# The product q (kᵀv) as two 64-row tiles of the TensorE array, in an fp32 attention + two-layer MoE kernel on one core

## The chip, the cores and the metric

The program runs on 1 core of one Trainium2 chip. Its time is the device time of that core in microseconds (us). It was timed three times before the change; "median" is the median of these. A further execution was recorded by the profiler, and all rows below are from it.

## The reference

Three blocks follow one another on 2304 tokens (4 batches of 576) and a width of 512 (8 heads of 64):

```python
kv  = einsum('bhsd,bhse->bhde', k, v)            # 64x64 per batch and head
out = einsum('bhsd,bhde->bhse', q, kv)
x   = out / sqrt(mean(out*out, -1) + 1e-6) * g_norm      # then heads side by side: x is [2304, 512]

h = x @ w_in ; x = (max(h,0) + alpha*min(h,0)) @ w_out    # d_ff 2048

P = exp(x @ w_gate - max) ; 8 times: rows / sum, columns / sum, * N/E
y = sum over 8 experts e of P[:, e] * (max(x @ w1[e], 0) @ w2[e])    # d_ff 1024 each
```

All inputs and the output are float32. The change lies wholly in the second einsum and what reads its result; it keeps the values.

## The kernel before, in words

Each of the five engines has an instruction list of its own, written out by hand; the order in a list is the order in time, and lists meet only at semaphores (`wait_ge`, `then_inc`). No planner is involved. TensorE is PE below, VectorE DVE, ScalarE ACT, GpSimd POOL, SyncE SP.

**Attention** is worked in 16 turns (`TURNS`), one for each batch and pair of heads (h = 0, 1). The 576 tokens of a turn lie as 96 partitions times 6 tokens (`ROWS`, `TG`), and are taken in pairs: an even token (o = 0) and the odd one after it (o = 1). For turn n:

- SP loads q, k and v (288 KB each) into one of four buffer sets (`load_qkv`, L352). From turn 4 on it first waits for `kv_done` of the turn four before. The weights of the first MoE unit are loaded behind turn 5, those of the next two behind turn 15 (L368, L373).
- PE `turn_q` (L926): 6 transposes bring q to qT, for each (h, t) a block of 128 rows (even token's 64 dimensions above, odd one's below) by 96 columns. ACT `take_q` (L502) copies it from PSUM.
- PE `multiply_kv` (L941): kᵀv, summed for even tokens in PSUM rows 0 to 63 and for odd ones in rows 64 to 127. Each of its 12 matmuls (24 instructions, since fp32 goes in two passes) loads 64 columns and moves 64: two halves of the array by columns. It waits for `kv_in` and for `kvd_ready` of the turn before.
- ACT `take_kv` (L507) copies the two halves to `kvp`; PE `spread_kv` (L948) multiplies by the matrix `both`, which adds the halves and leaves the sum in both; DVE `take_kv` (L690) copies it to `kvd`.
- PE `multiply_q` (L958), for turn n in the PE list behind `multiply_kv` of turn n+1: 6 matmuls (12 instructions), stationary the 128 x 96 block of qT, moving the 128 x 128 block of `kvd`. `kvd` is block diagonal: kᵀv in two corners, zeros in the other two, so one matmul gives the outputs of an even and of an odd token. The zeros are written once by POOL (L418).
- ACT `squares` (L512) and DVE `square_sums` (L683) sum squares over 64; ACT `root` (L517), DVE `norm` (L696 reciprocal, L700 multiply) give the normalised `xs`; PE `turn_x` (L972), two groups of 3 transposes, and ACT `take_x` (L523), twice, bring it to `x` with the factor g_norm.

The PE list of a turn is: `turn_q(n)`, `turn_x(n-3, 0)`, `multiply_kv(n)`, `turn_x(n-3, 1)`, `multiply_q(n-1)`, `spread_kv(n)`. Both halves of `turn_x` write one PSUM bank, so the second waits until ACT has copied the first. The ACT list of a turn is `squares(n-2)`, `take_q(n)`, `take_x(n-3, 0)`, `root(n-2)`, `take_kv(n)`, `take_x(n-3, 1)`. `multiply_q` of turn 15 and the last `turn_x` stand among the first matmuls of the MoE blocks (`behind`). In the last turns (13 to 15) DVE also runs `factor_low` (L726), which splits x for the MoE blocks.

**The MoE blocks** run in 120 units on the same five engines; matmuls in fp32r with the operands split in high and low parts (L1050, L1052, L1053 the first product, L1078 to L1080 the second). Nothing of them is touched by the change.

Of the kernel before, what the change touches and what calls it, by code (L numbers as in the profile page):

```python
# [8 lines left out]
ALU = mybir.AluOpType  # L9
ACT = mybir.ActivationFunctionType  # L10
AX_X = mybir.AxisListType.X

P = 128
BATCH, HEADS, SEQ, DH = 4, 8, 576, 64
# [7 lines left out]
ROWS = 96  # L22
TG = SEQ // ROWS
# [40 lines left out]
def moe_program(nc, q, k, v, g_norm, w_in, w_out, alpha, w_gate, w1, w2, out):  # L64
    ctx = ExitStack()
    with ctx:
        cursor = [(nc.sbuf_base + 31) // 32 * 32]

        def sb(name, shape, dt, at=None):

            size = 4
            for n in shape[1:]:
                size *= n
            where = cursor[0] if at is None else at
            if at is None:
                cursor[0] += (size + 31) // 32 * 32
                assert cursor[0] <= nc.sbuf_usable_end, (name, cursor[0], nc.sbuf_usable_end)
            return nc.alloc_sbuf_tensor_at(name, shape, dt, offset=where)

        def sem(name):  # L80
            return ctx.enter_context(nc.semaphore(name))
# [17 lines left out]
        hh_at = cursor[0]  # L99
# [30 lines left out]
        BUFFER = 2 * TG * DH * 4  # L130
# [5 lines left out]
        def attention_buffers(at, **shapes):  # L136
            found = []
            for name, shape in shapes.items():
                found.append(sb(name, shape, F32, at=at))
                at += (4 * math.prod(shape[1:]) + 31) // 32 * 32  # L140
            return found

        qT, xs, kvp = attention_buffers(acc_at, qT=[P, 2, SEQ], xs=[ROWS, 2, TG, 2, DH], kvp=[P, 2, DH])
        sq, ssq, rms, rinv = attention_buffers(hh_at + 4 * BUFFER, sq=[ROWS, 2, TG, DH], ssq=[ROWS, 2 * TG],
                                               rms=[ROWS, 2, 2 * TG], rinv=[ROWS, 2 * TG])
        kvd, = attention_buffers(hh_at + 4 * BUFFER + 4096 + 2 * BUFFER, kvd=[P, 2, 2, P])
        alpha_rows = c22[0:MLP_SETS * 2 * CHUNKS, 0:P]

        ps = ctx.enter_context(nc.psum_tensor("ps", [P, 8, 512], F32))

        const_ready = sem("const_ready")
# [11 lines left out]
        kvd_ready = sem("kvd_ready")  # L163
# [5 lines left out]
        xs_ready = sem("xs_ready")  # L169
# [139 lines left out]
        def o_banks(n):  # L309
            return ps[0:ROWS, 2 * (n % 2):2 * (n % 2) + 2, 0:TG * DH]  # L310
# [93 lines left out]
        def _(pool):  # L404
            made = [0]

            def constant(instruction):
                made[0] += 1
                instruction.then_inc(const_ready, 1)
                pool.wait_ge(const_ready, made[0])  # L410

            def diagonal(m, base):
                constant(nc.gpsimd.affine_select(out=m, in_=m, compare_op=ALU.not_equal, fill=1.0, base=base,
                                                 pattern=[[-1, P]], channel_multiplier=1))

            constant(nc.gpsimd.memset(ident[:, :], 0.0))
            diagonal(ident[:, :], 0)
            constant(nc.gpsimd.memset(kvd[:, :, :, :], 0.0))  # L418
            constant(nc.gpsimd.memset(both[:, :], 0.0))
            for base in (0, DH, -DH):  # L420
                diagonal(both[:, :], base)
# [71 lines left out]
        def _(sc):  # L493
# [15 lines left out]

            def squares(n):  # L510
                sc.wait_ge(o_done, n + 1)
                nc.scalar.activation(sq[:, :, :, :].rearrange("p h t d -> p h (t d)"), o_banks(n), ACT.Square)\  # L512
                    .then_inc(sq_ready, 1)

            def root(n):
# [15 lines left out]
                nc.scalar.activation(high(s, i), whole(s, i), ACT.Copy).then_inc(xc_hi, 1)  # L531


            sc.wait_ge(const_ready, 8)
            nc.scalar.activation(unused[:, :], eps[:, :], ACT.Sqrt).then_inc(table_in, 1)
            for n in range(TURNS):
                if n >= 2:
# [78 lines left out]
            def step(u):  # L616
                s = stage_of(u) + 1
                splits = SPLITS_AT.get(before_last(u), ())
                if u == 0:
                    squares(TAIL_X + 1)  # L620
                    take_x(TAIL_X, 0)
                    take_x(TAIL_X, 1)
# [57 lines left out]
        def _(dve):  # L680
            def square_sums(n):
                dve.wait_ge(sq_ready, n + 1)
                nc.vector.reduce_sum(ssq[:, :], sq[:, :, :, :].rearrange("p h t d -> p (h t) d"), AX_X)\  # L683
                    .then_inc(ssq_ready, 1)

            def take_kv(n):
                dve.wait_ge(kv_spread, n + 1)
                for o in range(2):
                    r = slice(o * DH, (o + 1) * DH)
                    last = nc.vector.tensor_copy(  # L690
                        kvd[r, n % 2, :, r], ps[r, 6, 2 * P:2 * P + 2 * DH].rearrange("d (h e) -> d h e", h=2))
                last.then_inc(kvd_ready, 1)

            def norm(n):
                dve.wait_ge(rms_ready, n + 1)
                nc.vector.reciprocal(rinv[:, :], rms[:, n % 2]).then_inc(rinv_ready, 1)  # L696
                dve.wait_ge(rinv_ready, n + 1)
                if n >= 2:
                    dve.wait_ge(x_turned, 2 * (n - 1))
                nc.vector.tensor_tensor(  # L700
                    xs[:, n % 2].rearrange("p t h d -> p h t d"),
                    o_banks(n).rearrange("p h (t d) -> p h t d", d=DH),
                    rinv[:, :].rearrange("p (h t) -> p h t", h=2).unsqueeze(3).to_broadcast([ROWS, 2, TG, DH]),
                    ALU.mult).then_inc(xs_ready, 1)

            def factor_sum(s, i):

# [94 lines left out]
            spread = [P, GT, EXPERTS]  # L802
# [92 lines left out]
                        nc.vector.tensor_scalar(acc[:, t, :], acc[:, t, :], gate[:, t, 0:1], None, ALU.mult)\  # L895
                            .then_inc(gated, 1)

            dve.wait_ge(const_ready, 3)
            for n in range(TURNS):
                if n >= 2:  # L900
                    square_sums(n - 2)
# [14 lines left out]
        def _(pe):  # L916

            def turn_q(n):
                b, i = divmod(n, HEAD_PAIRS)
                qq = qkv[i][0].rearrange("p h (s o) d -> p h s (o d)", o=2)  # L920
                pe.wait_ge(q_in[i], 16 * (b + 1))
                if n >= 1:
                    pe.wait_ge(qT_ready, n)
                for h in range(2):
                    for t in range(TG // 2):
                        last = nc.tensor.transpose(ps[:, 4 + h, t * ROWS:(t + 1) * ROWS], qq[:, h, t, :],  # L926
                                                   ident[0:ROWS, 0:ROWS])
                last.then_inc(q_turned, 1)
# [16 lines left out]
            def spread_kv(n):  # L945

                pe.wait_ge(kvp_ready, n + 1)
                nc.tensor.matmul(ps[:, 6, 2 * P:2 * P + 2 * DH], both[:, :], kvp[:, :, :].rearrange("d h e -> d (h e)"),  # L948
                                 start=True, stop=True).then_inc(kv_spread, 1)

            def multiply_q(n):
                pe.wait_ge(qT_ready, n + 1)
                pe.wait_ge(kvd_ready, n + 1)
                if n >= 2:
                    pe.wait_ge(xs_ready, n - 1)
                for h in range(2):
                    for t in range(TG // 2):
                        last = nc.tensor.matmul(o_banks(n)[:, h, t * P:(t + 1) * P],  # L958
                                                qT[:, n % 2, (3 * h + t) * ROWS:(3 * h + t + 1) * ROWS],
                                                kvd[:, n % 2, h, :], start=True, stop=True)  # L960
                last.then_inc(o_done, 1)

            def turn_x(n, j):
                pe.wait_ge(xs_ready, n + 1)
                if n < TAIL_X:
                    pe.wait_ge(x_ready, 2 * n + j)
                else:
                    pe.wait_ge(qT_ready, TURNS)
                    if n > TAIL_X:
                        pe.wait_ge(x_ready, 2 * (n - 1) + j + 1)  # L970
                for t in range(TG // 2):
                    last = nc.tensor.transpose(x_bank(n, j)[:, t * ROWS:(t + 1) * ROWS], xs[:, n % 2, TG // 2 * j + t].rearrange("p h d -> p (h d)"),  # L972
                                               ident[0:ROWS, 0:ROWS])
                last.then_inc(x_turned, 1)

            pe.wait_ge(const_ready, 2)
            for n in range(TURNS):
                if n == 2:
                    pe.wait_ge(small_in, 64)
                    a = MLP_SETS * 2 * CHUNKS  # L980
                    nc.tensor.transpose(ps[:, 7, 0:a], alpha_rows, ident[0:a, 0:a]).then_inc(alpha_t, 1)
                if n == 3:
                    pe.wait_ge(alpha_ready, 1)
                turn_q(n)
                if n >= 3:
                    turn_x(n - 3, 0)
                if n == 0:
                    pe.wait_ge(const_ready, 7)
                multiply_kv(n)
                if n >= 3:  # L990
                    turn_x(n - 3, 1)
                if n >= 1:
                    multiply_q(n - 1)
                spread_kv(n)
# [121 lines left out]
            for u in range(UNITS + 1):  # L1116
                for i in range(PRODUCTS):
# [6 lines left out]
                    at = turn_at(u, i)  # L1124
                    if at:
                        turn_x2(*at)
                    at = logits_at(u, i)
# [22 lines left out]
```

## Time and profile before

| | us |
|---|---|
| three runs | 1993.55, 1994.24, 1995.27 (median 1994.24) |
| the profiled execution | 1995.62 |
| its span, first to last instruction | 1993.8 |
| PE busy | 1973.4 (99%) |
| POOL busy | 1149.3 (58%) |
| ACT busy | 810.3 (41%) |
| DVE busy | 798.4 (40%) |
| DMA | 146.44 MB, mean 73 GB/s |

A row of a group of instructions gives the line of the kernel, the engine, what is written and read, the shape, the count, and the busy time with the mean of one in ns. PEld is PE's loading of the stationary operand, which runs beside its matmuls. Ends of matmuls are modelled, their starts are not; the duration of one includes the way through the array, so matmuls behind one another overlap, and what one costs is the distance of two starts. PEclk is the granted TensorE clock: 1.00 is 2.4 GHz, 0.50 is 1.2 GHz.

### The profile page before, as it was taken

Reading aid. Unit: us, or ns where it says so; the run is one execution under the profiler, and the core shown is the slowest. Engines: PE = TensorE matmul, PEld = TensorE weight load, DVE = VectorE, ACT = ScalarE, POOL = GpSimd, SP = SyncE. Lnnn points to the kernel's source line nnn. Section 1 sums busy time; section 2 is a strip of 40 time slices with the busy share of each in tenths; the row PEclk is TensorE's granted clock in tenths of the full one; section 3 lists DMA queues with packets and bytes.
Section 4 is the critical chain, followed back from the end, with each engine's and each line's share of the span. In section 5 each row is a group of like instructions: output and inputs, shape, how many; then the busy total and the mean of one; then the engine's idle time right before and its main releaser. Section 6 shows DMA issues by size and latency. Waiting matters only on the chain.

```text
span 1993.8 us, 26242 instructions
## 1 busy us (share of the span) xinstructions
PE 1973.4 (99%) x10396; PEld 1774.9 (89%) x10396; DVE 798.4 (40%) x1386; ACT 810.3 (41%) x1400; POOL 1149.3 (58%) x860
## 2 busy tenths in 40 slices
PE   8899999999999999999999999999999999999999
PEld 7888988988888898888888888988888888888888
DVE  4755556554454332334323333233432333323333
ACT  5644444444433333434434333344343343333432
POOL 2366466465556666556665566655666655666553
PEclk9999999999999999999999999999999999999999
DMA  9422222222222222222232222222223222222221
GB/s 253 108 64 64 64 64 64 64 64 64 64 64 64 64 65 77 71 64 64 64 107 74 64 64 63 69 80 64 64 64 96 81 68 64 64 64 75 74 64 43
DMA packets 174985, 146.44 MB, mean 73 GB/s; under 512 B 9728, under 2 KB 141840, under 8 KB 174864
## 3 DMA queue, kind: packets, MB, share of 16 engines
q1 hardware_dynamic: 174144, 144.74, 24.7%
q8 instruction: 83, 1.36, 0.3%
q14 instruction: 38, 0.31, 0.1%
q10 hardware_dynamic: 720, 0.03, 0.0%
HBM read 140.01 MB, written 4.72 MB: 73 GB/s over the span
## 4 chain that ended last, share of the span: by engine, by line
PE 96%; DVE 1%; DMA 1%; SPq 0%; issue 0%; ACT 0%; DVEq 0%
PE ps L1080 17%; PE ps L1079 17%; PE ps L1078 16%; PE ps L1052 15%; PE ps L1050 14%; PE ps L1053 14%; DMA qkv<-in_v 1%; PE ps L1094 1%; PE ps L958 1%; PE ps L941 1%; PE ps L1086 0%; PE ps L972 0%; DVE x_parts L726 0%; PE ps L926 0%; SPq L373 0%
## 5 line engine op out<-in xcount | busy, mean ns | idle before, releaser
L445 POOL TENSOR_TENSOR w1l<-raw,w1h 128x768 fp32r<-128x768 f32 x120 | 222.9, 1858 | 756.6 <-PE ps L1053 742.8
L1080 PE MATMUL ps<-w2h,hh 128*128 128x512 f32 x1440 | 571.6, 397 | 0.0
L1079 PE MATMUL ps<-w2l,hh 128*128 128x512 f32 x1440 | 568.7, 395 | 0.0
L1050 PE MATMUL ps<-ring_parts,w1h 128*128 128x384 f32 x1680 | 564.6, 336 | 3.6 <-DVE c L763 1.8
L1053 PE MATMUL ps<-ring_parts,w1l 128*128 128x384 f32 x1680 | 562.5, 335 | 0.0
L1078 PE MATMUL ps<-w2h,hh 128*128 128x512 f32 x1440 | 560.5, 389 | 0.0
L579 ACT ACTIVATE hh<-ps 128x384 fp32r<-128x384 f32 x240 | 118.3, 493 | 618.6 <-DVE ps L763 495.0
L1050 PEld LDWEIGHTS ps<-ring_parts,w1h 128*128 128x128 f32 x1680 | 316.4, 188 | 34.4 <-DVE x_parts L726 2.1
L1052 PE MATMUL ps<-x_parts,w1h 128*128 128x384 f32 x960 | 323.9, 337 | 0.0
L1080 PEld LDWEIGHTS ps<-w2h,hh 128*128 128x128 f32 x1440 | 269.8, 187 | 57.3
L1053 PEld LDWEIGHTS ps<-ring_parts,w1l 128*128 128x128 f32 x1680 | 316.2, 188 | 0.0
L1078 PEld LDWEIGHTS ps<-w2h,hh 128*128 128x128 f32 x1440 | 270.7, 188 | 34.2
L1079 PEld LDWEIGHTS ps<-w2l,hh 128*128 128x128 f32 x1440 | 269.8, 187 | 34.0
L456 POOL TENSOR_TENSOR w2l<-raw,w2h 128x1024 fp32r<-128x1024 f32 x120 | 288.4, 2403 | 8.1 <-ACT w2h L569 8.0
L449 POOL TENSOR_TENSOR w1l<-tt,w1h 128x1024 fp32r<-128x1024 f32 x120 | 289.1, 2409 | 1.2 <-ACT w1h L564 1.2
L752 DVE SCALAR_TENSOR_TENSOR hh<-ps,hh 128x384 fp32r<-128x384 f32 x288 | 160.7, 558 | 228.7 <-ACT hh L592 118.6
L1052 PE MATMUL ps<-ring_parts,w1h 128*128 128x384 f32 x720 | 242.7, 337 | 0.0
L1052 PEld LDWEIGHTS ps<-x_parts,w1h 128*128 128x128 f32 x960 | 181.1, 189 | 16.4
L763 DVE TENSOR_TENSOR c<-ps,m5s 128x384 f32<-128x384 f32 x120 | 66.9, 557 | 247.9 <-PE ps L1053 247.6
L763 DVE TENSOR_TENSOR ps<-ps,m1s 128x384 f32<-128x384 f32 x120 | 68.0, 566 | 235.5 <-PE ps L1053 235.5
L624 ACT ACTIVATE m1s<-ps 128x384 f32<-128x384 f32 x120 | 59.1, 493 | 242.9 <-PE ps L1053 242.9
L1052 PEld LDWEIGHTS ps<-ring_parts,w1h 128*128 128x128 f32 x720 | 135.2, 188 | 16.5
(100 smaller groups left out, 1786.3 us busy)
## 6 DMA issues: line engine op xcount, KB each, us to landing
raw<-in_moe_w SPq DMA_DIRECT2D x384, 256.0 KB, 3.4
raw<-in_moe_w_in SPq DMA_DIRECT2D x48, 256.0 KB, 3.9
raw<-in_moe_w_out SPq DMA_DIRECT2D x48, 256.0 KB, 3.0
qkv<-in_q SPq DMA_DIRECT2D x16, 288.0 KB, 9.2
qkv<-in_k SPq DMA_DIRECT2D x16, 288.0 KB, 7.7
qkv<-in_v SPq DMA_DIRECT2D x16, 288.0 KB, 10.2
out<-acc SPq DMA_DIRECT2D x12, 192.0 KB, 2.5
out<-acc SPq DMA_DIRECT2D x12, 128.0 KB, 2.4
```

Source lines behind the costliest of these rows:

```text
L445: nc.gpsimd.tensor_tensor(w1l[:, u % 2, B22:T1, :].rearrange("p m c -> p (m c)"), r[:, KW:4 * KW], w1h[:, u % 2, B22:T1, :].rearrange("p m ...
L449: nc.gpsimd.tensor_tensor(w1l[:, u % 2, T1:, :].rearrange("p m c -> p (m c)"), tt[:, :, :].rearrange("p m c -> p (m c)"), w1h[:, u % 2, T1 ...
L456: nc.gpsimd.tensor_tensor(w2l[:, u % 2].rearrange("p i d -> p (i d)"), raw2[:, u % 2].rearrange("p i d -> p (i d)"), w2h[:, u % 2].rearran ...
L579: nc.scalar.activation(hh[:, u % 2, 0, j, :], side_bank(u), ACT.Copy if mlp(u) else ACT.Relu)\
L752: return nc.vector.scalar_tensor_tensor(lo, src, 0.0, hi, ALU.max, ALU.subtract)
L763: nc.vector.tensor_tensor(dst, bank, add, ALU.add).then_inc(c_done, 1)
L1050: nc.tensor.matmul(bank, wh, xh, start=i in (M1, M2, M5) and kt == 0, stop=False, skip_group_check=True)
L1052: nc.tensor.matmul(bank, wh, xl, start=False, stop=False, skip_group_check=True)
L1053: last = nc.tensor.matmul(bank, wl, xh, start=False, stop=kt == KH - 1, skip_group_check=True)
L1078: nc.tensor.matmul(ps[:, t, :], hi, wh, start=opens_sum(u) and i == 0, stop=False)
L1079: nc.tensor.matmul(ps[:, t, :], hi, wl, start=False, stop=False)
L1080: last = nc.tensor.matmul(ps[:, t, :], lo, wh, start=False, stop=closes_sum(u) and i == 1)
```

## The change

`multiply_q` is made of 12 matmuls (24 instructions) in place of 6 (12): for each (h, t), one with the upper 64 rows of qT and of `kvd` (even token) and one with the lower 64 rows (odd token). Each loads 64 x 96 and moves 64 x 64. The even ones write one PSUM bank, the odd ones the other, both at rows 0 to 95. `kvd` holds no zero blocks: it is 128 x 64 for each head, DVE copies it in one instruction of all 128 partitions in place of two of 64, and POOL's memset of it is gone, with it one count of `const_ready` and DVE's wait for it. The order of the outputs in PSUM is (o, h, s) in place of (h, t): `squares` and `square_sums` only rename their dimensions; the multiply of `norm` is two instructions of 96 x 384 in place of one of 96 x 768, the semaphore on the last.

```diff
--- before.py
+++ after.py
@@ -143,7 +143,7 @@
         qT, xs, kvp = attention_buffers(acc_at, qT=[P, 2, SEQ], xs=[ROWS, 2, TG, 2, DH], kvp=[P, 2, DH])
         sq, ssq, rms, rinv = attention_buffers(hh_at + 4 * BUFFER, sq=[ROWS, 2, TG, DH], ssq=[ROWS, 2 * TG],
                                                rms=[ROWS, 2, 2 * TG], rinv=[ROWS, 2 * TG])
-        kvd, = attention_buffers(hh_at + 4 * BUFFER + 4096 + 2 * BUFFER, kvd=[P, 2, 2, P])
+        kvd, = attention_buffers(hh_at + 4 * BUFFER + 4096 + 2 * BUFFER, kvd=[P, 2, 2, DH])
         alpha_rows = c22[0:MLP_SETS * 2 * CHUNKS, 0:P]
 
         ps = ctx.enter_context(nc.psum_tensor("ps", [P, 8, 512], F32))
@@ -415,7 +415,6 @@
 
             constant(nc.gpsimd.memset(ident[:, :], 0.0))
             diagonal(ident[:, :], 0)
-            constant(nc.gpsimd.memset(kvd[:, :, :, :], 0.0))
             constant(nc.gpsimd.memset(both[:, :], 0.0))
             for base in (0, DH, -DH):
                 diagonal(both[:, :], base)
@@ -509,7 +508,7 @@
 
             def squares(n):
                 sc.wait_ge(o_done, n + 1)
-                nc.scalar.activation(sq[:, :, :, :].rearrange("p h t d -> p h (t d)"), o_banks(n), ACT.Square)\
+                nc.scalar.activation(sq[:, :, :, :].rearrange("p o s d -> p o (s d)"), o_banks(n), ACT.Square)\
                     .then_inc(sq_ready, 1)
 
             def root(n):
@@ -531,7 +530,7 @@
                 nc.scalar.activation(high(s, i), whole(s, i), ACT.Copy).then_inc(xc_hi, 1)
 
 
-            sc.wait_ge(const_ready, 8)
+            sc.wait_ge(const_ready, 7)
             nc.scalar.activation(unused[:, :], eps[:, :], ACT.Sqrt).then_inc(table_in, 1)
             for n in range(TURNS):
                 if n >= 2:
@@ -680,16 +679,13 @@
         def _(dve):
             def square_sums(n):
                 dve.wait_ge(sq_ready, n + 1)
-                nc.vector.reduce_sum(ssq[:, :], sq[:, :, :, :].rearrange("p h t d -> p (h t) d"), AX_X)\
+                nc.vector.reduce_sum(ssq[:, :], sq[:, :, :, :].rearrange("p o s d -> p (o s) d"), AX_X)\
                     .then_inc(ssq_ready, 1)
 
             def take_kv(n):
                 dve.wait_ge(kv_spread, n + 1)
-                for o in range(2):
-                    r = slice(o * DH, (o + 1) * DH)
-                    last = nc.vector.tensor_copy(
-                        kvd[r, n % 2, :, r], ps[r, 6, 2 * P:2 * P + 2 * DH].rearrange("d (h e) -> d h e", h=2))
-                last.then_inc(kvd_ready, 1)
+                nc.vector.tensor_copy(kvd[:, n % 2].rearrange("d h e -> d (h e)"), ps[:, 6, 2 * P:2 * P + 2 * DH])\
+                    .then_inc(kvd_ready, 1)
 
             def norm(n):
                 dve.wait_ge(rms_ready, n + 1)
@@ -697,11 +693,13 @@
                 dve.wait_ge(rinv_ready, n + 1)
                 if n >= 2:
                     dve.wait_ge(x_turned, 2 * (n - 1))
-                nc.vector.tensor_tensor(
-                    xs[:, n % 2].rearrange("p t h d -> p h t d"),
-                    o_banks(n).rearrange("p h (t d) -> p h t d", d=DH),
-                    rinv[:, :].rearrange("p (h t) -> p h t", h=2).unsqueeze(3).to_broadcast([ROWS, 2, TG, DH]),
-                    ALU.mult).then_inc(xs_ready, 1)
+                spread = rinv[:, :].rearrange("p (o h s) -> p o h s", o=2, h=2)
+                for o in range(2):
+                    last = nc.vector.tensor_tensor(
+                        xs[:, n % 2].rearrange("p (s o) h d -> p o h s d", o=2)[:, o],
+                        o_banks(n)[:, o].rearrange("p (h s d) -> p h s d", h=2, d=DH),
+                        spread[:, o].unsqueeze(3).to_broadcast([ROWS, 2, TG // 2, DH]), ALU.mult)
+                last.then_inc(xs_ready, 1)
 
             def factor_sum(s, i):
 
@@ -895,7 +893,6 @@
                         nc.vector.tensor_scalar(acc[:, t, :], acc[:, t, :], gate[:, t, 0:1], None, ALU.mult)\
                             .then_inc(gated, 1)
 
-            dve.wait_ge(const_ready, 3)
             for n in range(TURNS):
                 if n >= 2:
                     square_sums(n - 2)
@@ -949,15 +946,20 @@
                                  start=True, stop=True).then_inc(kv_spread, 1)
 
             def multiply_q(n):
+
+
                 pe.wait_ge(qT_ready, n + 1)
                 pe.wait_ge(kvd_ready, n + 1)
                 if n >= 2:
                     pe.wait_ge(xs_ready, n - 1)
                 for h in range(2):
                     for t in range(TG // 2):
-                        last = nc.tensor.matmul(o_banks(n)[:, h, t * P:(t + 1) * P],
-                                                qT[:, n % 2, (3 * h + t) * ROWS:(3 * h + t + 1) * ROWS],
-                                                kvd[:, n % 2, h, :], start=True, stop=True)
+                        for o in range(2):
+                            r = slice(o * DH, (o + 1) * DH)
+                            at = (3 * h + t) * DH
+                            last = nc.tensor.matmul(o_banks(n)[:, o, at:at + DH],
+                                                    qT[r, n % 2, (3 * h + t) * ROWS:(3 * h + t + 1) * ROWS],
+                                                    kvd[r, n % 2, h, :], start=True, stop=True)
                 last.then_inc(o_done, 1)
 
             def turn_x(n, j):
@@ -985,7 +987,7 @@
                 if n >= 3:
                     turn_x(n - 3, 0)
                 if n == 0:
-                    pe.wait_ge(const_ready, 7)
+                    pe.wait_ge(const_ready, 6)
                 multiply_kv(n)
                 if n >= 3:
                     turn_x(n - 3, 1)
```

## Rows read from the trace of the kernel before

**Rows 1.** The page, part 4: shares of the chain that ended last, by engine.
```profile
PE 96%; DVE 1%; DMA 1%; SPq 0%; issue 0%; ACT 0%; DVEq 0%
```
**Rows 2.** Windows: stretch, length, busy of PE, PEld, DVE, ACT, POOL, PEclk, DMA share, GB/s.
```profile
34.00:39.25 5.25, 5.18 (x50) 4.91 (x51) 1.67 (x5) 1.74 (x4) 5.17 (x4) 0.67 1.09 270
39.25:61.41 22.16, 21.84 (x300) 20.26 (x301) 16.21 (x31) 17.83 (x39) 9.05 (x5) 1.00 1.09 266
64.41:74.25 9.84, 8.00 (x107) 7.17 (x104) 8.90 (x16) 8.14 (x18) 3.58 (x4) 1.00 0.29 88
104.00:1993.00 1889.00, 1883.79 (x9489) 1692.99 (x9487) 734.82 (x1276) 750.18 (x1276) 1113.32 (x822) 1.00 0.23 68
```
**Rows 3.** Chain that ended last, pieces in order of time: start us, us, what.
```profile
22.51 11.49 DMA qkv<-in_v
...
40.64 1.31 PE ps L958 x12
41.95 0.22 PE ps L948 x2
42.17 0.50 PE ps L926 x6
42.67 0.25 PE ps L972 x3
42.95 0.92 PE ps L941 x24
43.89 0.44 PE ps L972 x3
```
**Rows 4.** Timeline of that turn, two copies of ACT: start us, us, what.
```profile
42.71 0.65 ACT L502 ACTIVATE qT<-ps 128x576 f32<-128x576 f32 x1
...
43.25 0.49 ACT L523 ACTIVATE x<-ps,gcol 128x288 f32<-128x288 f32 x1
```
**Rows 5.** Weight loads: lines L1094, L958 (ns min/median/max), and L1094's first by time.
```profile
L1094 PEld LDWEIGHTS ps<-wg,x x144: 188/192/193, 214.9 to 499.4; 128*128 128x128 f32 x144
L958 PEld LDWEIGHTS ps<-kvd,qT x72: 162/163/165, 40.4 to 60.0; 128*96 128x96 f32 x72
214.86 0.97 PEld L1094 LDWEIGHTS ps<-wg,x 128*128 128x128 f32 x8
```
**Rows 6.** Timeline of PE around 17.3 and 18.2 us (turn 2).
```profile
17.01 0.59 PE L926 MATMUL ps<-ident,qkv 96*128 96x96 f32 x3
17.53 0.28 PE L941 MATMUL ps<-qkv,qkv 96*64 96x64 f32 x2
17.98 0.46 PE L941 MATMUL ps<-qkv,qkv 96*64 96x64 f32 x10
18.37 0.35 PE L958 MATMUL ps<-kvd,qT 128*96 128x128 f32 x1
```
**Rows 7.** DMA issues from 54.9 to 56.2 us: count, size, us to landing.
```profile
qkv<-in_v SPq DMA_DIRECT2D x1, 288.0 KB, 7.3
```
**Rows 8.** Chain that ended last, 64.4 to 74 us, two of its DVE pieces.
```profile
64.67 0.29 DVE kvd L690
...
72.65 0.96 DVE xs L700
```
**Rows 9.** Groups by form, first 180 us, DVE: busy us, mean ns.
```profile
L700 DVE TENSOR_TENSOR xs<-ps,rinv 96x768 f32<-96x768 f32 x16 | 15.2, 953 | 0.8 <-DVE rinv L696 0.3
L690 DVE COPY kvd<-ps 64x128 f32<-64x128 f32 x32 | 9.2, 288 | 25.1 <-PE ps L948 24.9
L763 DVE TENSOR_TENSOR ps<-ps,m1s 128x384 f32<-128x384 f32 x7 | 4.0, 567 | 12.0 <-PE ps L1053 12.0
```
**Rows 10.** Windows around two stretches at half clock, columns as in rows 2.
```profile
30.80:34.10 3.30, 1.51 (x16) 1.14 (x15) 1.79 (x5) 2.03 (x4) 3.22 (x5) 1.00 1.10 264
34.43:37.84 3.41, 3.41 (x32) 3.29 (x28) 0.58 (x1) 0.78 (x2) 3.41 (x3) 0.50 1.07 268
85.60:92.40 6.80, 6.18 (x18) 5.73 (x19) 4.27 (x8) 1.43 (x3) 5.06 (x5) 0.50 0.24 72
```

## The prediction

> **What bounds the kernel now.** I read the page's chain of waits first: PE holds 96% of it [rows 1]. Then the windows, to see where PE is not alone. From 104 us to the end PE is busy 1883.79 of 1889 us [rows 2], so whatever the attention gains or loses before 104 us moves the end by the same amount, and nothing of the change is left to do there. The change acts on some 5% of the span, the first 104 us.
>
> In that part the chain shows four stretches, and the reader should see a different last waiter in each.
> Up to 34.04 us turn 6 waits for its v: the chain holds one load of 11.49 us from 22.51 [rows 3], and the DMA share is at 1.10 [rows 10]. PE is idle 1.8 of the 3.3 us before it [rows 10]. A faster or slightly slower turn changes nothing there.
> From 39.25 (turn 7's k^T v) to 61.41 (turn 13's), six turns of 22.16 / 6 = 3.69 us, PE is busy 21.84 of 22.16 [rows 2]. One turn in the chain: 1.31 `multiply_q`, 0.22 spread, 0.50 + 0.25 transposes, 0.92 k^T v with its tail, 0.44 with its tail for the second transposes, and rounding [rows 3]. Here `multiply_q` is wholly on the path.
> From 64.4 to 74.25 DVE sets the pace: busy 8.90 of 9.84 against PE's 8.00 [rows 2], its copies and multiplies stand in the chain [rows 8].
> Behind it the first MoE unit again hangs on DVE, and the clock is at half from 85.6 to 92.4 [rows 10].
>
> **The change, part by part.**
>
> *The matmuls.* Before: 12 steps of 1.31 / 12 = 0.109 us. After: 24 instructions, 12 for each tile. Three questions set their cost.
> What does a step cost a tile? It has a load of 96 columns and a move of 64. A move of 64 columns costs 0.058 us at most where two tiles run: k^T v needs 24 instructions in 0.92 less one matmul's tail of 0.22, that is 0.70, 0.058 a pair. The load is longer: where the move is short (8 columns), loads of 128 columns follow one another at (0.97 - 0.19) / 7 = 0.111 us [rows 5]; the 96-column load is recorded 0.029 us shorter than the 128-column one (163 against 192 ns) [rows 5], so 0.082, or by columns 0.111 x 96 / 128 = 0.083. I take 0.084: a step is bound by its load, not its move, because the stationary side stays 96 columns wide while the moving side is halved.
> Do the two tiles load side by side? No row shows row tiles. The nearest are the column tiles of k^T v: 0.029 us an instruction, where one 64-column load alone would be 0.111 / 2 = 0.056. So they load in pairs, and I take the same for rows: 12 x 0.084 = 1.01 us, a gain of 0.30. Bounds: if loads were free, 12 x 0.058 = 0.70 (gain 0.61); if they went one behind the other, 24 x 0.084 = 2.02 (loss 0.71).
> What does the change of tiles cost? In turn 2 nothing but the array is waited for. The last transpose starts at about 17.60 - 0.26 = 17.34 and the first k^T v matmul at 17.53: 0.19 us, where neighbours of one kind are 0.50 / 6 = 0.08 apart. On the way back: last start 18.44 - 0.22 = 18.22, next 18.37, 0.15 in place of 0.03 [rows 3, 6]. So each change of tiling costs 0.11 to 0.12. The new `multiply_q` stands between full-array transposes and the full-array spread and has two of them per turn: 0.23. Bounds: nothing, if only column tiles need it, to 0.4 (a whole tail of 0.2 each).
>
> The Trainium skill ("TensorEngine Tiling (Array Packing)", Tiling Modes, Key Properties) says that changing the tiling mode, as against changing tile, drains TensorE. The trace has it for column tiles, with the 0.11 and 0.12 above; for row tiles no run here shows it yet.
>
> Is the path still PE's? The second transposes wait for ACT's copy of the first: q's copy starts at 42.71, 0.04 after the transposes of q end (42.01 + 0.66), the x copy 0.54 later, 43.25 + 0.49 = 43.74, and PE's chain goes on at 43.89 [rows 3, 4]. q's transposes follow the spread, which follows `multiply_q`, so this side road is as long as PE's own and shifts by the same amount, the exit drain included. Therefore the shorter wait for `kvd` (below) gives nothing here.
> Per turn: -0.30 + 0.23 = -0.07 us. Six turns: -0.4. Turn 6 to 7 runs mostly at half clock (0.67 mean) [rows 2]; both terms about double, -0.1.
> If PE did get much faster, DMA would be next: the last v, issued at 55.82, lands 7.3 us later, at 63.1 [rows 7], while k^T v of turn 15 starts at 69.45. It carries 884.7 KB a turn at 266 GB/s [rows 2], 3.3 us. At 3.62 us a turn it stays hidden.
>
> *`kvd` in one copy.* Two of 0.288 [rows 9] become one of 128 partitions with the same 128 elements each, 0.29: -0.29 a turn on DVE. *`norm` in two multiplies.* 953 ns for 768 elements and 567 for 384 [rows 9] give 2 x 0.56 = 1.12, +0.16 a turn. Bounds: nothing (overlapping starts) to +0.25. Both lie beside PE in the steady turns (DVE busy 16.21 of 22.16 [rows 2]). In the DVE stretch the chain has two such copies of turns 13 and 14 and two such multiplies [rows 8]: -0.56 + 0.32 = -0.24. In the first MoE unit one more multiply is in DVE's list before the value that PE waits for at 85.6: +0.16. `multiply_q` of turn 15 stands there between products whose next waits are on DVE; its two drains are covered by that.
>
> *The memset of 0.5 us and the waits on it.* POOL and DVE wait for data then; PE's first k^T v waits for v at 7.8 us. Nothing. The squares read the same number of elements: nothing.
>
> **Sum:** -0.4 - 0.1 - 0.24 + 0.16 = -0.6 us. The profiled execution of 1995.62 would be 1995.0; it lies 1.4 above the median of 1994.24, so the forecast for the median is 1993.7. A change below 0.2% (4.0 us) can't be told from none by a measurement of this kernel.
>
> **The rivals.**
>
> 1. *The tiles give the full gain.* The step is paced by the move, 0.058 a pair: -0.61 + 0.23 = -0.38 a turn, -2.3 for six, -0.5 for the half-clock turn, -0.1 for the rest: 1991.3. Without the drains DMA's 3.3 us a turn would cap it near 1991. For it: k^T v does reach 0.058, with loads as wide as moves. Against: here loads are half again as wide as moves. The Trainium skill ("TensorEngine Tiling (Array Packing)", Theoretical Speedup) gives up to twice the throughput for a contraction of 64 or less, which is this rival; this trace has twice the rate for column tiles only.
>
> 2. *Slower: the tiles' loads go one behind the other.* Place: `multiply_q` in every turn. 2.02 + 0.23 against 1.31, +0.94 a turn. It decides once the 1.8 us of PE's idle time before 34.04 [rows 10] is used: three turns bring +2.8, so +1.0 there, +1.9 for the half-clock turn, 6 x 0.94 = 5.6 up to turn 13: +8.5, 2002.7. For it: no row shows row tiles loading together. Against: column tiles do, though they read the same partitions, and row tiles read different ones. The milder form (loads hidden, moves one after another, 24 x 0.058 = 1.39) gives +0.31 a turn, +2.3: 1996.5, still no measurable change.
>
> 3. *Slower: the clock.* It was at half from 34.43 to 37.84, after 1.8 us of idle time in 3.3, and from 85.6 to 92.4 [rows 10]. `multiply_q` keeps half of the array's rows and half of the columns moved at a time, so the array may look less active. Each further stretch of 3.41 us at half clock costs at most 1.7. One or two leave the result within 4 us (1995 to 1997); if it stayed down through the PE-bound turns, each would lose some 2.7: up to +15, 2009. Nothing of the trace shows a fall during the steady turns.
>
> 4. *Faster beyond 4 us.* The half-clock stretch at 85.6, worth up to 3.4 us, shortens because the wait before it moves, on top of rival 1: about 1989.5.
>
> **How the numbers follow.** My forecast 0.53 (own range 1991.8 to 1995.2); rival 1 0.13; rival 2 0.09, its mild form 0.08; rival 3 0.12, of which 0.06 over 4 us; rival 4 0.05. Slower by over 0.2%: 0.09 + 0.06 = 0.15. Faster: 0.05. Same: 0.80. The range 1990.0 to 2000.0 leaves out rival 2's full form, the long form of 3 and most of 4, just under 0.2.
>
> **What would show it.** In the changed kernel's steady turns: L958's successors as 24 matmuls whose starts span about 1.0 us (0.7: rival 1; 1.3: its mild slower form; 2.0: rival 2); gaps of 0.19 and 0.15 before and behind them; a pitch of the turns of 3.62; ACT's x copy still just ahead of the second transposes. One `kvd` copy of 0.29 and two multiplies of 0.56. The same or nearly the same half-clock stretches. Wrong would be a pitch above 3.75, DMA landings that PE waits for after 39 us, or a clock below 1.00 between 39 and 61 us.

## The result

| | us |
|---|---|
| changed kernel, 5 runs | 2027.15 to 2029.52, median 2028.13 |
| kernel before, 5 runs beside it | 1993.55 to 1995.51, median 1994.24 |
| ratio | 1.0165, 95% interval 1.0153 to 1.0176 |

The change made the kernel 34 us slower (1.65%). The forecast was 1993.7, with a range up to 2000.0.

The page of the changed kernel, its first lines (busy us, share of the span, instructions):

```profile
span 2026.6 us, 26624 instructions
PE 2010.4 (99%) x10588; PEld 1806.1 (89%) x10588; DVE 793.6 (39%) x1386; ACT 812.4 (40%) x1400; POOL 1148.5 (57%) x859
```

First, where. A window as long as the last of [rows 2], laid from 137 us to 2026 us (stretch, length, busy of PE, PEld, DVE, ACT, POOL, clock, DMA share, GB/s), has PE busy 1883.61 us with 9488 matmuls, against 1883.79 us with 9489. The whole difference lies before it. The first matmul of the second MoE product (128 x 512) starts at 92.45 us before and at 125.2 after, 32.7 later; the end is 32.8 later.

```profile
42.27:80.87 38.60, 38.60 (x373) 34.50 (x373) 14.31 (x30) 17.62 (x38) 7.25 (x4) 1.00 0.54 143
137.00:2026.00 1889.00, 1883.61 (x9488) 1692.85 (x9486) 734.74 (x1275) 750.31 (x1276) 1113.58 (x822) 1.00 0.23 68
```

Second, what. Six turns of the attention, from turn 6's k^T v to turn 12's, are the first of these windows: 38.60 us, 6.43 a turn, where [rows 2] had 22.16, 3.69 a turn. PE is busy all of it, DMA's share is half of what it was (0.54 for 1.09), and DVE is busy 14.31 of 38.60. The chain of waits of one turn (start us, us, what), against [rows 3]:

```profile
42.34 1.48 PE ps L938 x24
43.82 0.67 PE ps L974 x3
44.49 2.12 PE ps L960 x24
46.61 0.72 PE ps L945 x2
47.33 0.96 PE ps L923 x6
48.29 0.48 PE ps L974 x3
```

The reader should look at the pieces that the change did not touch. q's transposes take 0.96 where they took 0.50, the next three 0.48 for 0.25, k^T v 1.48 for 0.92. What the change left alone takes 1.6 to 1.9 times its time: the clock is at half. The column PEclk shows 1.00 in the window above, but that is no reading: the record has no change of clock before 108 us and the column is filled with 1.00 up to the first one. It is the distance of like matmuls that tells. In this timeline of PE (start us, us, what) one product's matmuls start 0.31 to 0.33 apart up to 108.28 and 0.17 to 0.19 apart behind it:

```profile
107.00 0.52 PE L1052 MATMUL ps<-ring_parts,w1h 128*128 128x384 f32 x1
107.33 0.52 PE L1054 MATMUL ps<-x_parts,w1h 128*128 128x384 f32 x1
...
108.47 0.34 PE L1055 MATMUL ps<-ring_parts,w1l 128*128 128x384 f32 x1
108.65 0.34 PE L1052 MATMUL ps<-ring_parts,w1h 128*128 128x384 f32 x1
```

In the kernel before the record has the first rise at 17.36 us, among the last transposes of turn 2. One `multiply_q`, that of turn 0, had run by then, at half clock; that of turn 1 starts at 18.37 us. The start of the two kernels (start us, us, what), before and then after:

```profile
13.03 2.88 PE L958 MATMUL ps<-kvd,qT 128*96 128x128 f32 x12
16.48 1.12 PE L926 MATMUL ps<-ident,qkv 96*128 96x96 f32 x6
17.53 0.92 PE L941 MATMUL ps<-qkv,qkv 96*64 96x64 f32 x24
```

```profile
13.00 2.19 PE L960 MATMUL ps<-kvd,qT 64*96 64x64 f32 x24
16.06 1.22 PE L923 MATMUL ps<-ident,qkv 96*128 96x96 f32 x6
17.21 1.55 PE L938 MATMUL ps<-qkv,qkv 96*64 96x64 f32 x24
```

k^T v takes 0.92 us at 17.53 in the first and 1.55 at 17.21 in the second. The tiled kernel missed the rise and ran its attention at 1.2 GHz, all but `multiply_q` of turn 15.

Third, the change itself at full clock. `multiply_q` of turn 15 comes after the rise (line, durations in ns min/median/max, first and last start; then the same by time: start us, us):

```profile
L960 PEld LDWEIGHTS ps<-kvd,qT x24: 156/162/162, 109.3 to 110.2; 64*96 64x96 f32 x24
L960 PE MATMUL ps<-kvd,qT x24: 245/245/293, 109.3 to 110.3; 64*96 64x64 f32 x24
```

```profile
109.26 1.24 PE L960 MATMUL ps<-kvd,qT 64*96 64x64 f32 x24
```

1.24 less one matmul of 0.245 is 1.00 from first start to last: the 1.01 of the forecast. On DVE the two multiplies are 548 ns each and the one copy 292 (groups by form, first 200 us), forecast 560 and 290 [rows 9]:

```profile
L698 DVE TENSOR_TENSOR xs<-ps,rinv 96x384 f32<-96x384 f32 x32 | 16.3, 548 | 0.6
L687 DVE COPY kvd<-ps 128x128 f32<-128x128 f32 x16 | 4.7, 292 | 54.8 <-PE ps L945 54.8
```

So the question of the runs is what of the change holds the clock down.

### The profile page after: what moved, and what is told of

It reads as the page before. It is cut to its first block, busy times and chain, and to the rows that moved or that the text cites. A ratio compares the mean times of both kernels' runs of the same rounds, so it can differ in the third digit from the quotient of the medians.

```text
span 2026.6 us, 26624 instructions
## 1 busy us (share of the span) xinstructions
PE 2010.4 (99%) x10588; PEld 1806.1 (89%) x10588; DVE 793.6 (39%) x1386; ACT 812.4 (40%) x1400; POOL 1148.5 (57%) x859
## 4 chain that ended last, share of the span: by engine, by line
PE 98%; DVE 1%; DMA 0%; issue 0%; ACT 0%; SPq 0%; DVEq 0%
PE ps L1082 17%; PE ps L1081 16%; PE ps L1080 16%; PE ps L1054 14%; PE ps L1052 14%; PE ps L1055 14%; PE ps L960 2%; PE ps L938 1%; PE ps L974 1%; PE ps L1096 1%; PE ps L923 1%; PE ps L945 1%; DMA qkv<-in_v 0%; PE ps L1088 0%; DVE acc L893 0%
```

## Experiments

In all of them the kernel before ran beside the others on the same chip, with medians of 1994.5 to 1995.6 us.

Three theories of why the clock stays at half are named by letters in the recorded expectations. A: the attention turns of the changed kernel keep too little of the array at work. B: the row tiling itself holds the clock down. C: only the rise at 17 us was missed, and once up the clock would stay.

**Tiles that move 128 columns.** Same tiles, same number of instructions, same changes of tiling; only the moved side is as wide as before. (`kvd` is one block longer and is set to zero at the start, as before the change; `multiply_q` of turn 0 still starts at 12.96 us, against 13.00.)

```diff
-    last = nc.tensor.matmul(o_banks(n)[:, o, at:at + DH], qT[r, ...], kvd[r, n % 2, h, :], ...)
+    last = nc.tensor.matmul(ps[0:ROWS, 2 * (n % 2) + o, at:at + 2 * DH], qT[r, ...],
+                            kvd[r, n % 2, h:h + 2, :].rearrange("d h e -> d (h e)"), ...)
```

> The changed kernel with every tile of multiply_q moving 128 columns in place of 64 (both heads' blocks; the second 64 results are overwritten or never read). Tiles, drains and instruction count stay as in the change, the moved columns per tile double. A expects the clock up in the attention: multiply_q 12 x 0.109 = 1.31 us, turns of 3.69 + 0.23 = 3.92 us, 1995 to 1998 us. B expects half clock: turns of 6.43 + 0.6 = 7.0 us, 2034 to 2040 us.

Measured: 1997.91 us (1994.37 to 1999.83, 10 runs), ratio 1.0011, interval 1.0002 to 1.0020. Windows of this run:

```profile
34.54:66.00 31.46, 30.74 (x486) 26.84 (x487) 18.62 (x38) 22.99 (x50) 13.76 (x8) 1.00 1.10 257
88.80:95.50 6.70, 5.29 (x16) 5.03 (x17) 3.98 (x9) 0.98 (x2) 3.66 (x5) 0.50 0.01 3
```

Here the column can be read, since the record has a rise at 17.1 us and no fall before 88.8: full clock through the attention. Doubling the moved columns, which is more work, takes back 30 of the 34 us. Row tiling and its changes of mode are therefore not what holds the clock down: theory B falls.

**The kernel before with half the columns.** No tiles at all; `multiply_q` loads as before and moves 64 columns. The odd tokens' outputs are left out and stay zero, set once by DVE at the start.

```diff
-    last = nc.tensor.matmul(o_banks(n)[:, h, t * P:(t + 1) * P], qT[...], kvd[:, n % 2, h, :], ...)
+    last = nc.tensor.matmul(o_banks(n)[:, h, t * P:t * P + DH], qT[...], kvd[:, n % 2, h, 0:DH], ...)
```

> The kernel before, untiled, but multiply_q moves only the even tokens' 64 columns of the block-diagonal right side (the odd tokens' outputs are left out and stay zero, set once by DVE at the start). Full height, 12 instructions, no tile mode in it, load-bound as the tiles are, and as many rows times columns at work as in the changed kernel. If the clock goes by how much of the array works (A1 or A2), it doesn't rise at 17 us and stays at half for all or most of the attention: turns of about 6 us, 2012 to 2028 us. If the row tiling holds it down (B), the clock rises as before: 1990 to 1994 us.

Measured: 2021.94 us (2021.45 to 2022.84, 4 runs), ratio 1.0136, interval 1.0120 to 1.0151. The untiled kernel, moving half as much in `multiply_q`, stays at half clock: the first rise on record is at 101.2 us. `multiply_q` of two steady turns, one behind the other (start us, us, what):

```profile
48.39 2.07 PE L962 MATMUL ps<-kvd,qT 128*96 128x64 f32 x12
...
54.38 2.07 PE L962 MATMUL ps<-kvd,qT 128*96 128x64 f32 x12
```

The turn is 5.99 us, 0.44 less than the tiled kernel's 6.43; the two changes of tiling that the forecast put at 0.23 would be 0.46 at half clock. These two runs together narrow it down: of what the change did to `multiply_q`, it is the halving of what is moved that costs the clock, with tiles or without. They don't separate the columns from the length of the block, which shrinks with them: at half clock turn 0's takes 2.88 us before and 2.19 after, and 2.70 in a kernel with wide tiles (the wide start below).

**Fillers in each turn.**

```diff
+    for _ in range(3):
+        nc.tensor.matmul(ps[:, 2 * (n % 2), 0:P], both[:, :], both[:, :], start=True, stop=True)
     for h in range(2):
```

> The changed kernel with 3 full-array 128 x 128 fp32 matmuls (6 instructions) in each turn ahead of multiply_q, into the bank that it then overwrites. They give back the 768 moved full-height columns per turn that the tiles took away. A expects the clock to come up as in the kernel before, turns of 3.62 + 0.66 = 4.3 us, about 1999 to 2001 us, faster than the changed kernel though it does more. B expects half clock still: turns of 6.43 + 1.3 = 7.8 us, about 2048 us. C is undecided.

Measured: 2028.8 us, four runs from 2013.36 to 2040.71, ratio 1.0164, interval 1.0102 to 1.0226. Neither theory's number. The profiled run has turns of 7.77 us at half clock up to 76.4 us and then, without a fall in the attention, 4.44 us:

```profile
65.19 1.55 PE L938 MATMUL ps<-qkv,qkv 96*64 96x64 f32 x24
...
72.96 1.55 PE L938 MATMUL ps<-qkv,qkv 96*64 96x64 f32 x24
...
83.21 0.92 PE L938 MATMUL ps<-qkv,qkv 96*64 96x64 f32 x24
...
87.65 0.92 PE L938 MATMUL ps<-qkv,qkv 96*64 96x64 f32 x24
```

The columns of a turn add up to those of the kernel before, and still the rise comes late. The four results lie up to 27 us apart, so the rise probably comes at another time in each; only one run was profiled. The sum over a turn is therefore not the whole of it, and why fillers do less than the wide `multiply_q` stays open.

**A warm start.**

```diff
+    if n == 0:
+        for _ in range(16):
+            nc.tensor.matmul(ps[:, 7, 0:P], ident[:, :], ident[:, :], start=True, stop=True)
     turn_q(n)
```

> The changed kernel with 16 full-array 128 x 128 fp32 matmuls (32 instructions, identity by identity into a PSUM bank nobody uses then) ahead of turn 0's transposes. Three theories of why the changed kernel's TensorE stays at half clock until 108 us. A: the attention turns keep too little of the array at work, since multiply_q moves 64 columns per tile where it moved 128 over the whole array. B: the row tiling itself (tile mode, its drains) holds the clock down. C: only the rise at 17 us was missed, and once up the clock would stay. C expects full clock from about 11 us on, turns of 3.6 us, and 1993 to 1998 us in all. A and B expect the clock to rise for a short stretch and to fall back in the turns, turns of 6.4 us, and 2026 to 2033 us.

Measured: 2023.61 us (2018.56, 2019.29, 2027.93, 2028.63), ratio 1.0141, interval 1.0116 to 1.0166. Windows of the profiled run:

```profile
6.20:30.00 23.80, 20.66 (x343) 18.06 (x342) 10.30 (x22) 12.47 (x28) 2.62 (x4) 1.00 1.10 267
30.10:98.20 68.10, 67.43 (x633) 60.53 (x634) 28.59 (x56) 34.72 (x70) 19.39 (x15) 0.50 0.56 149
```

The clock rose at 6.2 us and held through five tiled `multiply_q` (turns 0 to 4), and then it was down for 68 us, PE busy 67.43 of them; it rose again at 98.3 us, among the 128 x 384 products of the MoE blocks. The fall followed waits for loads and one stall within `multiply_q`:

```profile
26.91 0.38 PE L960 MATMUL ps<-kvd,qT 64*96 64x64 f32 x3
28.58 1.07 PE L960 MATMUL ps<-kvd,qT 64*96 64x64 f32 x21 [1.30 <-issue]
```

C is half right (the missed rise) and half wrong (being up once is not enough). It suggested a sharper form: the narrow turns keep a clock that they have, but can't bring one back.

**Warmed when no load is waited for.** The same 16 fillers ahead of turn 7.

> The changed kernel with 16 full-array 128 x 128 fp32 matmuls (32 instructions) ahead of turn 7's transposes, when the loads have run ahead and no turn waits for DMA any more. It asks whether the tiled turns keep a full clock once they have it. Theory A1 (the tiled turns work too little of the array to keep it): it rises in the fillers, falls within a turn or two, and the time is the changed kernel's plus up to 7 us, 2030 to 2036 us. Theory A2 (they work too little of the array only to raise it, and a fall needs a real gap): full clock from turn 7 on, turns of 3.6 us, about 2012 to 2016 us.

Measured: 2010.12 us (2008.71 to 2011.94, 4 runs), ratio 1.0075, interval 1.0062 to 1.0089: the case that the text on record calls A2, and 2 us better than its 2012 to 2016. Seven turns in one window, all at full clock (the record has the rise at 50.5 us), and the chain of one turn:

```profile
52.78:78.97 26.19, 25.31 (x435) 22.47 (x434) 16.77 (x35) 21.00 (x46) 9.01 (x7) 1.00 0.90 239
```

```profile
56.59 0.85 PE ps L938 x24
57.44 0.13 issue
57.57 0.44 PE ps L974 x3
58.01 1.16 PE ps L960 x24
59.17 0.42 PE ps L945 x2
59.59 0.50 PE ps L923 x6
60.09 0.25 PE ps L974 x3
```

That is 3.75 us; over seven turns 26.19 / 7 = 3.74. Against [rows 3] the piece of `multiply_q` is 0.15 shorter and that of the spread 0.20 longer. The forecast had 3.62, so the two changes of tiling cost about 0.12 more than taken. The timeline shows where. First PE around the spread, then the two loads of the spread here, and those of the kernel before:

```profile
61.68 1.24 PE L960 MATMUL ps<-kvd,qT 64*96 64x64 f32 x24
62.84 0.49 PE L945 MATMUL ps<-kvp,both 128*128 128x128 f32 x2
63.17 0.66 PE L923 MATMUL ps<-ident,qkv 96*128 96x96 f32 x6
```

```profile
62.84 0.30 PEld L945 LDWEIGHTS ps<-kvp,both 128*128 128x128 f32 x2
```

```profile
41.68 0.30 PEld L948 LDWEIGHTS ps<-kvp,both 128*128 128x128 f32 x2
```

The last tiled matmul starts at 61.68 + 1.24 - 0.25 = 62.67, the spread 0.17 later, near the forecast's 0.15. But the spread's loads begin with its first matmul, at 62.84, where the kernel before has them 0.11 ahead of it (41.68 and 41.79), and the transposes start 0.33 behind the spread in place of 0.22. After the change of tiling the first load was not made beside earlier matmuls, and that is the second 0.11.

**Tiles kept at full clock.** The changed kernel with fillers at the start (16), in turns 4, 5 and 7 (3 each) and 6 (14), and 9 and 3 of 128 x 384 in two waits of the first MoE unit.

> The changed kernel with full-array filler matmuls, results unused: 16 at the start, 3 in turns 4, 5 and 7 and 14 in turn 6, where it waits for loads, 9 and 3 in the two waits of the first MoE unit. If the fall to half clock is the whole loss of the change, it is now within 0.2% of the kernel before: turns of 3.74 us as in the run that was warmed at turn 7, no half-clock stretch at 30 or 85 us, 1990 to 1995 us. If something else of the change costs too, it stays above 2000 us.

Measured: median 2000.8 us, eleven of twelve runs from 1993.75 to 2011.51; one took 4574 us, which nothing here explains. Ratio 1.0032, interval 1.0017 to 1.0046. This is neither of the two outcomes on record. The profiled run lost its clock from 21.3 to 34.9 us, behind a wait of 1.59 us for v, then kept it: five turns from 48.80 to 67.51 us are 18.71 us long, 3.74 each.:

```profile
21.30:34.90 13.60, 13.60 (x124) 12.58 (x123) 4.85 (x11) 4.89 (x11) 6.50 (x8) 0.50 1.11 268
48.80:67.51 18.71, 18.08 (x311) 16.05 (x310) 12.41 (x26) 14.84 (x33) 7.24 (x4) 1.00 0.97 247
```

Of the eleven runs the slower ones have the lower mean clock (0.988 at 2011.51, 0.999 at 1993.75), so the fillers did not keep the clock up in each of them.

**Wide tiles in turns 0 and 1 only**, without fillers, and the same with 14 fillers in turn 6.

```diff
+    w = 2 if n < 2 else 1
-    ... ps[0:ROWS, 2 * (n % 2) + o, at:at + 2 * DH] ... kvd[r, n % 2, h:h + 2, :]
+    ... ps[0:ROWS, 2 * (n % 2) + o, at:at + w * DH] ... kvd[r, n % 2, h:h + w, :]
```

> The changed kernel with tiles of 128 columns in turns 0 and 1 only (second half unread), 64 columns from turn 2 on, no fillers. It tests the account 'narrow turns keep a clock but don't raise it' against 'narrow turns lose it by themselves'. By the first: full clock from about 17 us, narrow turns of 3.74 us at it, then either a fall at turn 6's wait for its loads (31 to 34 us) and half clock to the end of the attention, about 2018 to 2022 us, or, if the wait is short enough, none and 1995 to 1998 us. By the second: a fall before 30 us, 2024 us or more.

> The same with 14 full-array 128 x 128 fp32 fillers ahead of turn 6's k^T v. By the first account the clock stays up through turn 6's wait and the whole attention: 1994 to 1998 us, the tiled kernel level with the one before. By the second 2024 us or more.

Measured: the first 1998.47 us, ratio 1.0057, interval 1.0016 to 1.0098. Its ten runs stand in two groups with nothing between: six from 1993.29 to 1998.50, mean clock 0.997 to 0.999, and four from 2019.21 to 2022.56, mean clock 0.981 or 0.982. These are the two outcomes that the first account named. Here the only difference to the changed kernel that bears on the clock is the width of two turns out of sixteen. The profiled run, 1996.84 us, is of the fast group. Its clock rose at 15.37 us, within the wide `multiply_q` of turn 0, and stayed up to 73.4 us, through 13 narrow ones (turns 2 to 14) and several short idle stretches, the longest of them 0.83 us:

```profile
15.40:73.30 57.90, 52.47 (x873) 45.59 (x870) 37.53 (x76) 42.81 (x91) 22.14 (x18) 1.00 1.01 245
```

No run of the slow group was profiled. Its mean clock of 0.982 over 2018 us is about 73 us at half clock, against 10 in the profiled run; that fits a fall near turn 6 and half clock to the end of the attention, but where the fall came is an inference.

The second took 1999.48 us, ratio 1.0044, interval 1.0018 to 1.0070, seven runs up to 2004.29 and three at 2014 to 2015. The fillers did not make it safe; in its profiled run the fall came later, at 52.8 us, right behind a stall of 2.40 us in which the engine waited for nothing that the profile shows:

```profile
48.53 0.46 PE L963 MATMUL ps<-kvd,qT 64*96 64x64 f32 x5
51.40 1.06 PE L963 MATMUL ps<-kvd,qT 64*96 64x64 f32 x19 [2.40 <-issue]
52.39 0.49 PE L947 MATMUL ps<-kvp,both 128*128 128x128 f32 x2
52.72 1.12 PE L925 MATMUL ps<-ident,qkv 96*128 96x96 f32 x6
```

Behind it transposes are at 1.12 for six in place of 0.66, and they stay so for 41 us. The kernel before comes back after its gap at 34 us within 3.4 us [rows 10]; here the clock is back at 93.7 us only, among the products of the MoE blocks, and in the warm start likewise. A fall needs not follow each stall: the first kernel of the next experiment stood for 1.41 us without one.

**The kernel before with fillers.** Does it lose anything to its own gaps? 6 fillers in turn 6's wait, 8 and 3 in the first MoE unit; then once more with the first MoE unit's (9 and 3) placed ahead of the wait they are to fill.

> The kernel before with filler matmuls, results unused, in three of TensorE's waits: 6 of 128 x 128 fp32 in the wait for turn 6's v (idle 1.8 of 3.3 us there), 8 of 128 x 384 fp32r ahead of the product that waits until 85.6 us, 3 ahead of the next one at 88.5. If the falls to half clock at 34.4 and 85.6 come from these gaps, both vanish: 1.7 + 3.4 us less, 1989 to 1991 us. If a fill only delays, 1995 to 1997 us. If the clock rises and falls on its own, 1994 to 1996 us.

> The kernel before with 6 fillers in turn 6's wait for v, and those of the first MoE unit placed at the head of the wait that ends at 85.6 us (9 of 128 x 384) and 3 at 88.5. [...] Expected: no half clock after the first rise, 1990 to 1992.5 us if the gaps are the cause of the falls; 1993 to 1994 us if the stall comes again; 1995 us if the fillers only delay.

Measured: 1993.83 us, ratio 0.9995 (0.9987 to 1.0004), and 1994.01 us, ratio 0.9992 (0.9984 to 1.0001). In both profiled runs the half-clock stretches of [rows 10] are gone, so the gaps are their cause:

```profile
84.00:91.00 7.00, 5.64 (x31) 5.14 (x31) 6.14 (x10) 3.13 (x6) 5.49 (x6) 1.00 0.26 75
```

```profile
18.10:92.00 73.90, 68.62 (x799) 63.15 (x798) 55.67 (x98) 49.99 (x106) 29.36 (x24) 1.00 0.77 189
```

(a window of the first kernel, then one of the second). In the first PE stood for 1.41 us ahead of the spread at 56.18 us, waiting for nothing that the profile shows; that is the stall that the second expectation reckons with. What they win is 1 to 1.6 us, not 5, and the interval holds 1. The first is the fastest of all versions by its median, but its gain can't be told from none by these runs. Both lie above what was expected if the gaps are the cause (1989 to 1991 and 1990 to 1992.5), though the half-clock stretches went.

## Why the prediction was wrong

- *Where the time is decided.* Right: the long stretch behind the first MoE unit kept its length, and what was lost before it came out at the end, 32.7 of 32.8.
- *A step is bound by its load; the two tiles work side by side.* Right: 1.00 us against 1.01 for the block at full clock. Rivals 1 and 2 and the mild form of 2 fall. The Trainium skill ("TensorE: Matmul & The Clock Gate", Part 3: Packing small matmuls — row/col tiling, The mechanism) says under "What overlaps and what doesn't" that a load overlaps matmuls in flight only where the row groups differ; the paragraph above it also allows a load into the background weight buffer. By the first sentence alone a step of one tile would be load and move, 0.085 + 0.058, and the block 1.7 us, an estimate from this case's rows. The trace agrees with the second: 0.085 a step is the load alone (0.084 in the forecast), so loads were made beside matmuls of the same rows.
- *Two changes of tiling, 0.23 a turn.* Right in kind, too small: the start after a change was taken, but not that on the way out the spread's first load comes late as well, 0.11 us. A turn at full clock is 3.74, not 3.62; with it the forecast would have been about 1994.6 (six turns at 0.12, the half-clock one at 0.24). One of the forecast's two readings, 17.34 to 17.53 in turn 2, lies across the rise of the clock at 17.36, so that its 0.11 is good by luck; the other, 0.12 at 18.22, is wholly at full clock, and the 0.17 measured bears it out.
- *DVE's two edits.* Right, 548 and 292 ns.
- *The clock.* This is the step that failed: the sum has no term for it. The forecast took it that the changed kernel would be at full clock through the steady turns, put 0.12 on rival 3, and gave as its reason that nothing of the trace shows a fall during them. That is true, and the wrong question: the clock had to rise first. The kernel starts at half clock. The forecast says nothing of the first 17 us, for which the column shows 1.00, though the matmuls there are at half speed: in the trace before, six transposes take 1.17 us at 10.40 and 0.66 at 19.98. The rise at 17.36 us followed the only `multiply_q` run by then, 12 matmuls of 128 columns in 2.88 us, and the change halves just what these move; the changed kernel had no rise up to 108.28 us. Rival 3 named the right cause, the halved work of the array, and its price of +2.7 for a turn at half clock was right (measured 6.43 - 3.69 = 2.74), but it priced a clock that falls and stays down through the six PE-bound turns only: +15, 2009. With the clock never up, all turns paid. k^T v starts 2.1 us later in turn 3, 8.2 in turn 6, where the 1.8 us of idle time were long used, 25.9 in turn 13, and 30.7 in turn 15, since the DVE-bound turns 13 to 15 were bound by PE too. Of the forecast's own signs of being wrong two came, a pitch above 3.75 (6.43) and half clock between 39 and 61 us, the second unseen in the column that it named.
- *Shown and not shown.* Shown: the halved move of `multiply_q`, not the tiling, costs the rise (tiles of 128 columns rise at 17.1 us, untiled 64 columns not before 101.2). The narrow turns can keep a full clock: 58 us in the profiled wide start, and in the kernel warmed at turn 7 from 52 us to the first MoE product at 87.6. After a fall they stayed at half clock to the end of the attention in the two profiled runs where that happened without fillers behind it (the warm start, the wide start with fillers in turn 6). Not settled: why fillers that restore the sum of columns raise it only late and irregularly, which gap makes it fall, and why the removed half-clock stretches of the kernel before give back a third or less of their price.

## What to carry to other kernels

Check, after an edit that makes TensorE move less, that the clock still rises where it did, and don't count only what each instruction costs at full clock. Here the columns taken away were useless ones, the zeros of a block-diagonal operand; without them the clock did not rise in the attention, and its turns took 6.43 us in place of 3.69. Read the clock from the distances of equal matmuls, since the column says nothing ahead of the first recorded change. Splitting this block into row tiles with loads as wide as before shortened it by little (1.31 to 1.00 us), and the way in and out took it back (0.15 won, 0.20 lost a turn).

## What the runs showed of the hardware

- Two row tiles of 64 do run side by side: 24 fp32 instructions of 96 loaded and 64 moved columns in 1.00 us, 0.085 for a pair of steps.
- At half clock with PE busy 67.43 of 68.10 us the clock did not come up in the warm start, nor with 38.60 of 38.60 in the changed kernel: a busy PE was not enough there.
- Once up, the clock stayed at full for 58 us of the same narrow turns, with PE busy 52.47 of 57.90 us.
- The same program can end in two groups 20 us apart (six runs below 1999, four above 2019, with mean clocks of 0.997 and more and of 0.982 and less).
- TensorE stood still, waiting for nothing that the profile shows, for 1.30 and 2.40 us within one block of tiled matmuls (the warm start, the wide start with fillers) and for 1.41 us ahead of a spread (the untiled kernel with fillers), each time with the DMA share at 1.1. What it waits for was not tried.
